# Attention, gated MLP and routed experts on one core: values of the second group fetched before two weight pieces, and two MLP slots in each of the first two steps

## What is computed

```python
# attention: batch 4, 8 heads, 576 tokens, head size 64
scores = scale * q @ k.T + bias            # ALiBi bias, causal, window of 128
attn = softmax(scores); x = attn @ v       # -> x: 2304 tokens x 512
# MLP: 512 -> 2048 -> 512
h = x @ w_in
y = (h * clip(h + 3, 0, 6) / 6) @ w_out
# experts: 8 of 512 -> 1024 -> 512, one for each token
expert_idx = argmax(cosine(y, expert_emb) / tau); gate_w = its probability
out[mask] = gate_w[mask] * (relu(y[mask] @ w1[e]) @ w2[e])
```

## Time and profile before

| | |
|---|---|
| median of 3 runs | 841.08 us (840.48 to 842.05) |
| profiled execution, its own time | 840.72 us |
| its span in the profile | 838.9 us |
| mean granted TensorE clock | 0.997 |
| TensorE matmul busy | 825.4 us (98%) |
| TensorE weight load busy | 707.9 us (84%) |
| VectorE, ScalarE, GpSimd busy | 477.3, 395.8, 242.0 us |

### The profile page before, as it was taken

One profiled execution on the slowest core, in us unless ns is written; L12 is line 12 of the kernel. 1 busy time (PEld: TensorE's weight loads), 2 busy tenths in 40 slices (PEclk: granted clock), 3 DMA queues, 4 the chain that ended last, 5 costly groups with the idle time before them and its releaser, 6 DMA issues.

```text
span 838.9 us, 18744 instructions
## 1 busy us (share of the span) xinstructions
PE 825.4 (98%) x6536; PEld 707.9 (84%) x6536; DVE 477.3 (57%) x1469; ACT 395.8 (47%) x1057; POOL 242.0 (29%) x261
## 2 busy tenths in 40 slices
PE   7999999999999999999999999999999999999996
PEld 6888888888888888888888988878888888888885
DVE  7765575665766656756565577775543445554000
ACT  4775555545455455554554336533434334343342
POOL 5992000000000000000000102386665655666432
PEclk9999999999999999999999999999999999999998
DMA  8764212102112111121100026565545444541100
GB/s 239 220 199 151 74 50 63 33 14 77 52 39 70 33 39 52 52 76 36 34 10 3 26 82 173 168 222 174 156 158 181 128 139 141 163 156 66 50 14 11
DMA packets 54428, 80.20 MB, mean 96 GB/s; under 512 B 11752, under 2 KB 28136, under 8 KB 54210
## 3 DMA queue, kind: packets, MB, share of 16 engines
q1 hardware_dynamic: 50050, 67.58, 26.3%
q0 software_dynamic: 4000, 11.29, 4.0%
q10 hardware_dynamic: 288, 0.13, 0.1%
HBM read 69.51 MB, written 11.30 MB: 96 GB/s over the span
## 4 chain that ended last, share of the span: by engine, by line
PE 94%; DMA 3%; DVE 1%; issue 1%; ACT 0%; SPq 0%; POOL 0%; POOLq 0%; ACTq 0%; DVEq 0%
PE ps_h L832 24%; PE ps_y L849 22%; PE ps_h L983 16%; PE ps_s L1012 15%; PE ps_out L777 4%; PE ps_s L740 3%; PE ps_y L1007 2%; DMA y_scratch<-gate_tok 2%; PE ps_out L1012 1%; PE ps_out L936 1%; PE ps_s L759 1%; PE ps_s L765 1%; PE ps_s L762 1%; DMA en_all<-y_scratch,gather_ids 1%; PE ps_out L901 0%
## 5 line engine op out<-in xcount | busy, mean ns | idle before, releaser
L832 PE MATMUL ps_h<-x_hi,win_hi 128*128 128x256 f32 x576 | 165.6, 295 | 0.1
L832 PE MATMUL ps_h<-x_lo,win_hi 128*128 128x256 f32 x576 | 158.5, 283 | 0.0
L832 PE MATMUL ps_h<-x_hi,win_lo 128*128 128x256 f32 x576 | 158.3, 283 | 0.0
L1400 DVE TENSOR_TENSOR gated_lo<-gated,gated_hi 128x256 fp32r<-128x256 f32 x144 | 66.6, 463 | 100.9 <-ACT gated_hi L1136 100.4
L1136 ACT CAST gated_hi<-gated 128x256 fp32r<-128x256 f32 x144 | 58.5, 406 | 137.0 <-PE ps_y L849 98.1
L832 PEld LDWEIGHTS ps_h<-x_hi,win_hi 128*128 128x128 f32 x576 | 107.8, 190 | 8.3 <-issue 2.7
L849 PE MATMUL ps_y<-wout_hi,gated_hi 128*128 128x512 f32 x288 | 114.1, 396 | 0.0
L849 PE MATMUL ps_y<-wout_hi,gated_lo 128*128 128x512 f32 x288 | 113.8, 395 | 0.0
L613 POOL MEMSET arena<- 128x64 bf16 x2 | 0.2, 151 | 390.9 <-DVE x_lo L1374 390.9
L849 PE MATMUL ps_y<-wout_lo,gated_hi 128*128 128x512 f32 x288 | 112.1, 389 | 0.0
L832 PEld LDWEIGHTS ps_h<-x_hi,win_lo 128*128 128x128 f32 x576 | 107.9, 191 | 2.3
(11 more groups left out here) (234 smaller groups left out, 1563.1 us busy)
## 6 DMA issues: line engine op xcount, KB each, us to landing
arena<-in_moe_w SPq DMA_DIRECT2D x64, 512.0 KB
arena<-in_v SPq DMA_DIRECT2D x40, 128.0 KB, 3.2
y_scratch<-y_sb SPq DMA_DIRECT2D x9, 512.0 KB, 3.7
en_all<-in_moe_w_in SPq DMA_DIRECT2D x16, 256.0 KB, 3.7
arena<-in_v SPq DMA_DIRECT2D x16, 256.0 KB, 3.3
en_all<-in_moe_w_out SPq DMA_DIRECT2D x16, 256.0 KB, 4.2
arena<-in_q SPq DMA_DIRECT2D x31, 128.0 KB, 2.4
arena<-in_k SPq DMA_DIRECT2D x31, 128.0 KB, 2.8
```

The costliest lines, as they stand in the source:

```text
L832: last = pe.matmul(ps_h[m % 2][:, 0:TB], a[:, c, w], r[:, c, x], start=n == 0, stop=n == 3 * KC - 1)
L1400: dve.tensor_tensor(gl[m % 2][:], gate[:], gh[m % 2][:], ALU.subtract).then_inc(dve_gl, 1)
```

## The change

```diff
@@ the planner of slots
-        begun.append(max(begun[-1], min(spare, pace, begun[-1] + 4)))
+
+        begun.append(max(begun[-1], min(spare, pace, begun[-1] + (2 if it < FIRST + 2 else 4))))
@@ SyncE, start
             for n in range(4):
                 sp.dma_start(w_raw[n], w_piece(n)).then_inc(ld_w[n], 16)
                 if n == 0:
                     load_v(0)
                     load_qk(4)
-            load_v(1)
+                if n == 1:
+                    load_v(1)
@@ TensorE, iterations 3 and 4
                 if 2 < it < FIRST:
-                    keep_busy((3, 14)[it - 3])
+                    keep_busy((3, 6)[it - 3])
                     values(it - OUT)
```

## The result

The changed kernel takes 845.11 us (median of 6 runs, 843.89 to 846.47), the kernel before beside it 840.78 (6 runs). The ratio is 1.005, with a 95% interval of 1.004 to 1.006: 4.3 us slower, where 4.8 was forecast. The profiled execution took 846.47 us, the longest of the six, with a span of 844.7. Of its 5.8 us more span 1.1 lies ahead of values(2), where the first values landed late (values(0) waited 0.94 us for them), and that belongs to this execution: in a second profile of the changed kernel values(2) began at 17.23. 4.9 lies between values(2) and values(9). Behind values(9) TensorE runs the same 5577 matmuls as before and is busy 740.06 us, where it was 740.00.

What follows compares the result with a forecast made beforehand. TensorE was taken to bound the kernel, with only the first 35 us movable. Pauses of 1.96 (the transposes' gain included) and 0.8 us plus 2.0 for the clock made +4.8 on 841.08: 845.8 us, range 843.0 to 847.8.

Steps and rivals of the forecast that it cites:

- Part 1: Step 4, ahead of values(2): eight transposes fewer take 0.87 us off the path.
- Part 2: First loads: group 1's values ahead of weight pieces 2 and 3; no gain, hidden cost, up to 2.8 us without cover.
- Part 3: Two slots each in steps 5 and 6: pauses ahead of values(4) and values(5), 1.96 + 0.8 = +2.76 us.
- The owed slot: Slot moved out of step 5, to be run later: costs 2.82 us, less 0.86 for reaching values(4) sooner.
- The second pause: Step 6, TensorE idle between transposes(5) and values(5): +0.8 us, bounds 0 and 1.5.
- Part 4: Behind the 3.4 us pause ahead of values(4): TensorE's clock halves for 4 us, +2.0 us, between 0 and 3.0.
- The sign of the 128x256 matmuls: Behind values(4): matmuls of 128x256 would take about twice 0.12 us each if the forecast was right.
- (b): Ahead of values(4): the pause comes but the clock holds, 843.8 us, between 843.0 and 844.6; chance 0.24.
- (c): Between transposes(4) and values(4): ScalarE copies early, TensorE hardly pauses; not slower, 840.2 us; chance 0.12.
- (d): Weights late: GpSimd's splits slip by more than 2.8 us, or engines wait; 847 to 849 us; chance 0.06.

Runs made afterwards that it cites:

- the old planner: Kernel before with group 1's values loaded early and 6 transposes instead of 14, slots 3, 4, 3, 4 kept: 842.85 us, ratio 1.0027.
- planner only: Kernel before with only the new slot order, 2, 2, 4, 4 slots: 845.72 us, ratio 1.006.
- two then four: Changed kernel with 2 slots in step 5 and 4 in step 6: 848.48 us against 842.89 for the kernel before, ratio 1.0062.
- values late: Changed kernel with group 1's values back behind weight piece 3, its other two parts kept: 847.80 us, ratio 1.0058 to the kernel before.
- the copy sooner: Changed kernel with ScalarE's copy of pT(4) ahead of slot 1's exponentials and clip: 843.59 us against 842.89 for the kernel before, ratio 1.001.
- fewer transposes alone: Kernel before with only 6 transposes instead of 14 ahead of values(2): 840.93 us against 840.65, ratio 0.9998.
- three then two slots: Changed kernel with 3 slots in step 5 and 2 in step 6: 844.01 us against 842.89 for the kernel before, ratio 1.0014.

## Why the prediction was right

**Part 1**, 0.87 us on the path: shown in the profiles (2.27 us to 1.42, that is 0.85); medians can't tell it. values(2) began at 20.06 and 17.23 in the two profiles of the changed kernel, not at 18.1 as the sign was put: the first loads move the start by more than the gain, and only the distance from transposes(2) tests this part.

**Part 2**, no gain, no cost behind the cover, up to 2.8 without it: right, and the cover is the planner's. GpSimd's chain slipped by 2.7 us at piece 2 and 2.0 at piece 11, inside the 1.1 to 2.8 given. With the old planner TensorE waited 0.69 and 1.50 us at up(4). One thing I had too low: in this profile the three issues took 2.53 us instead of 1.58, so piece 2 was issued 2.3 us later rather than 1.6. That belongs to the execution and not to the change: in the second profile of the changed kernel they took 1.58, and in the second one of before the three of the pieces took 2.69, where they had taken 1.43. For the late piece 1 it is open whether the transfers behind it slow it: GpSimd began it 6.45 us after its issue here and 4.93 in the second profile, and over all profiles 4.2 to 6.5 with the values early (nine) and 3.8 to 5.0 with the values late (five).

**Part 3**, from values(2) to values(4) 11.59 us forecast, 11.58 measured, with a pause of 3.4 forecast and 3.22 measured. The owed slot, 2.82 forecast, is 13.84 - 11.01 = 2.83 us, the distance from values(5) to values(6) with four slots in the step and with three. The second pause: +0.8 forecast, 0.60 of idle time, and 0.67 came back when it was removed.

**Part 4**, +2.0 us for the clock, between 0 and 3.0: ahead of values(4) it was lowered in each of the five profiles with a pause of 3.21 to 3.58 us (the change twice, planner only, two then four, values late) and stayed up with 1.08, as it did with 1.79 ahead of values(5). It cost 1.4 to 1.5 us; half of the 3.3 us of work at half rate would be 1.6. My 2.0 came from 4 us of work at half rate at the kernel's start and was 0.5 too large. The sum of the measured terms is 2.83 + 0.60 + 1.40 - 0.85 = 4.0 us, where I had 2.82 + 0.8 + 2.0 - 0.86 = 4.8; the measured difference, 3.4 to 5.0 us by its interval, fits both. That the clock would fall at all was less sure than the five profiles make it look: a wait of 3.14 us elsewhere left it up (last section). The sign of the 128x256 matmuls could not be read, since the first of them began at 34.61 and the clock was back at 34.9; values(4) and the scores behind them show the half rate instead.

Of the rivals, (b) fell with the clock rows; (c) fell because the copy did stand behind both slots, and the run with the copy sooner shows the mechanism: it shrank the pause and handed part of it to the next step; (d), late weights, is real with the old planner but not in the changed kernel.

No version beat both kernels: the best, fewer transposes alone, is level with the kernel before.

## What to carry to other kernels

Where an engine is busy all the time, look at what it does while another one reads its last result: the slot behind the transposes was not spare work but the cover of ScalarE's copy. With it or without it values(4) began 11.58 us after values(2), so moving it cost its whole 2.8 us later on. A pause of TensorE can also cost after it has ended, here 1.4 us, so price the clock with it. And test the parts together as well as alone: the early loads cost 1.6 us with the old order of slots and nothing that showed with the new.

## What was not expected

The expert stage has a wait of its own that comes and goes. In some executions, of the kernel before as well, TensorE waits 3.1 to 4.0 us for the first gathered rows, which stand behind the store of the gates: that store landed after 12.6 us in the first profile of before and after 14.8 in the second. In six of the seven profiles with such a wait the clock then falls in mid-kernel as it does behind values(4); in the second profile of before its mean over 520 to 525 us is 0.66, where it had been 1.00. In the seventh, three then two slots, TensorE waited 3.14 us, until 523.85, and the clock stayed up:
```profile
520.00:525.00 5.00, 4.14 (x13) 3.40 (x14) 0.62 (x2) 1.79 (x5) 1.98 (x2) 0.66 0.24 65
```
```profile
520.00:525.00 5.00, 1.86 (x11) 1.31 (x10) 2.70 (x3) 2.53 (x4) 2.98 (x3) 1.00 0.59 171
```
So the length of the wait alone does not decide: 3.07 us lowered the clock in the first of these two and 3.14 did not in the second. What does decide, no run shows. The pair gives the price of the drop once more. From values(9) to the end the first profile of before has 748.2 us, this one of three then two 750.9 and the second one of before 752.3: 2.8 us for the wait, and 1.4 for the clock.

With the clock, the wait is nearly as large as the change. It may explain much of the scatter on the second chip (841.4 to 847.8 for the kernel before), but only the profiled executions show it. Why the store lands later was not tried.
